# Attention unit: value products ahead of the carried-state matmuls, second masks ahead of the chain of states

## The reference, cut to what matters

```
B, H, S, D = 4, 8, 768, 48
for t in range(S):
    state = alpha[:, :, t, :, None] * state + einsum('bhd,bhe->bhde', k[:, :, t], v[:, :, t])
    y[:, :, t] = einsum('bhd,bhde->bhe', q[:, :, t], state)
```

## Time and profile before

| | before |
|---|---|
| median of 3 runs | 848.24 us |
| lowest, highest | 847.78, 849.92 us |
| profiled execution: span from first to last instruction (its own whole time is not shown) | 845.8 us |
| mean granted TensorE clock in it | 0.976 |
| TensorE busy | 784.4 us, 93% |
| VectorE busy | 409.7 us, 48% |
| ScalarE busy | 255.1 us, 30% |
| GpSimd busy | 268.3 us, 32% |

### The profile page before, as it was taken

One profiled execution on the slowest core, in us unless ns is written; L12 is line 12 of the kernel. 1 busy time (PEld: TensorE's weight loads), 2 busy tenths in 40 slices (PEclk: granted clock), 3 DMA queues, 4 the chain that ended last, 5 costly groups with the idle time before them and its releaser, 6 DMA issues.

```text
span 845.8 us, 15211 instructions
## 1 busy us (share of the span) xinstructions
PE 784.4 (93%) x4644; PEld 670.4 (79%) x4645; DVE 409.7 (48%) x735; ACT 255.1 (30%) x555; POOL 268.3 (32%) x170
## 2 busy tenths in 40 slices
PE   2988898989938999999999999999999999999998
PEld 2766676767726999999999987688888888888887
DVE  6788888888567334343333423433333333333322
ACT  5344636346232222222222222332222212122110
POOL 3245434352013745671826757410000001000000
PEclk9799999999878999999999999999999999999999
DMA  9966887845065814533325010210101101000001
GB/s 143 250 94 86 139 105 128 102 62 106 1 230 179 331 48 178 180 118 121 133 100 195 28 40 29 85 29 19 37 19 39 38 19 47 10 27 9 9 20 47
DMA packets 128881, 75.74 MB, mean 90 GB/s; under 512 B 102648, under 2 KB 122112, under 8 KB 128832
## 3 DMA queue, kind: packets, MB, share of 16 engines
q1 hardware_dynamic: 119632, 54.88, 30.0%
q0 software_dynamic: 3328, 10.23, 3.8%
q10 hardware_dynamic: 5872, 10.03, 3.2%
HBM read 59.00 MB, written 16.12 MB: 89 GB/s over the span
## 4 chain that ended last, share of the span: by engine, by line
PE 83%; DVE 11%; issue 2%; SPq 2%; DMA 1%; ACT 0%; POOL 0%; DVEq 0%; ACTq 0%
PE bank L1334 62%; DVE UA L834 4%; PE bank L1226 3%; DVE A L789 3%; PE bank L1136 3%; PE bank L1370 3%; PE bank L1196 2%; PE bank L1216 2%; PE bank L1166 2%; PE bank L1219 2%; SPq L300 2%; PE bank L1183 1%; PE bank L1320 1%; DVE UA L827 1%; PE bank L1406 1%
## 5 line engine op out<-in xcount | busy, mean ns | idle before, releaser
L465 POOL TENSOR_TENSOR wsp<-raw,wsp 128x1536 f32 x28 | 103.8, 3729 | 93.1 <-DVE wsp L1028 93.1
L1334 PE MATMUL bank<-yh,mh 128*128 128x512 f32 x324 | 128.3, 396 | 0.6 <-ACT yh L720 0.6
L1334 PE MATMUL bank<-yh,ml 128*128 128x512 f32 x324 | 126.5, 390 | 0.0
L1334 PE MATMUL bank<-yl,mh 128*128 128x512 f32 x324 | 91.3, 390 | 0.0
L1334 PE MATMUL bank<-wsp,xh 128*128 (+1 forms) x324 | 85.3, 399 | 3.7 <-issue 3.1
L1334 PE MATMUL bank<-wsp,hTh 128*128 x432 | 81.5, 340 | 1.1 <-ACT hTh L677 1.1
L506 POOL DMA_INDIRECT yg<-expert_rows,pos_i x24 | 24.7, 1029 | 171.8 <-ACT ygs L714 164.9
L1334 PEld LDWEIGHTS bank<-wsp,hTh 128*128 128x128 f32 x432 | 73.6, 188 | 1.3 <-issue 1.3
L1334 PEld LDWEIGHTS bank<-wsp,xh 128*128 128x128 f32 x324 | 58.9, 188 | 16.2 <-issue 4.0
L1098 DVE TENSOR_TENSOR t<-bank,tm 128x512 f32<-128x512 f32 x36 | 24.9, 692 | 96.5 <-PE bank L1334 96.5
L1334 PEld LDWEIGHTS bank<-yl,mh 128*128 128x128 f32 x324 | 60.9, 188 | 12.9
(11 more groups left out here) (197 smaller groups left out, 1394.8 us busy)
## 6 DMA issues: line engine op xcount, KB each, us to landing
raw<-in_moe_w SPq DMA_DIRECT2D x16, 1536.0 KB, 8.1
expert_rows<-ye ACTq DMA_DIRECT2D x27, 192.0 KB, 2.2
nat<-in_alpha SPq DMA_DIRECT2D x32, 144.0 KB, 3.1
nat<-in_k SPq DMA_DIRECT2D x32, 144.0 KB, 3.8
nat<-in_q SPq DMA_DIRECT2D x32, 144.0 KB, 4.3
vt<-in_v SPq DMA_DIRECT2D x32, 144.0 KB, 4.6
attention_rows<-xc SPq DMA_DIRECT2D x4, 1152.0 KB, 6.0
out<-oo SPq DMA_DIRECT2D x24, 192.0 KB, 1.9
```

What stands on the lines that cost most here:

```text
L465: g.tensor_tensor(wsp[:, ds(to, 1), 1, n, part], raw[:, n:n + 1, part], wsp[:, ds(to, 1), 0, n, part].bitcast(f32), ALU.subtract).then_inc ...
L1334: last = mm(o, x, y, start=(n == 0), stop=(n == len(todo) - 1))
```

## The change: value products, then carried states; second masks, then the chain

On TensorE all value products of a half are issued together (first half, then second half), each half behind its waits for masks and the keys' scaling. Then the five state matmuls follow, for chunks 1 to 5, each with its own wait, and add to what lies in PSUM. `pe_Y` is signalled behind the matmuls of chunk 2 and of chunk 5. On VectorE the two second masks are issued between the scans and the state products; they leave the chain.

```diff
@@ states (VectorE) @@
                 d.scalar_tensor_tensor(UA[j % 2][:, c, :], UA[j % 2][:, c - 1, :],
                                        A[j][:, P * c + P - 1:P * c + P], UA[j % 2][:, c, :],
                                        ALU.mult, ALU.add).then_inc(dve_st, 1)
-                if c <= 2:
-
-                    mask(u, j, 1, c - 1)
@@ step (VectorE) @@
             if base + j + 2 < NU:
                 scans(u + 2, (j + 2) % UPB)
+            for hd in range(2):
+                mask(u, j, 1, hd)
             states(u, j)
@@ unit (TensorE) @@
+            out = lambda cc: bank[2 + cc // HC][:, P * (cc % HC):P * (cc % HC) + P]
             for h in range(2):
                 if more:
                     pe.wait_ge(dve_kp, CR + 2 * (u + 1) + h + 1)
                 else:
                     pe.wait_ge(act_yT, CR + 2 * (u - 1) + h + 1)
                 pe.wait_ge(dve_S, CR + 4 * u + 2 * h + 2)
-                for c in range(HC):
-                    cc = HC * h + c
-                    o = bank[2 + h][:, P * c:P * c + P]
-                    if cc:
-
-                        pe.wait_ge(*((dve_UA, CR + u + 1) if cc == 1 else (dve_st, CR + 4 * u + cc - 1)))
-                        mm(o, UA[j % 2][:, cc - 1, :], qp[j % 2][:, P * cc:P * cc + P],
-                           start=True, stop=False, skip_group_check=True)
+
+                for cc in range(HC * h, HC * h + HC):
                     for hd in range(2):
-                        last = mm(o[HL * hd:HL * hd + HL], vt[j][:, cc, hd, :], Sm[j % 2][:, hd, cc, :],
-                                  start=not cc, stop=True, skip_group_check=True)
-                last.then_inc(pe_Y, 1)
+                        mm(out(cc)[HL * hd:HL * hd + HL], vt[j][:, cc, hd, :], Sm[j % 2][:, hd, cc, :],
+                           start=(cc == HC * h), stop=(cc == 0), skip_group_check=True)
+            for cc in range(1, CH):
+                pe.wait_ge(*((dve_UA, CR + u + 1) if cc == 1 else (dve_st, CR + 4 * u + cc - 1)))
+                last = mm(out(cc), UA[j % 2][:, cc - 1, :], qp[j % 2][:, P * cc:P * cc + P],
+                          start=False, stop=True, skip_group_check=True)
+                if cc in (HC - 1, CH - 1):
+                    last.then_inc(pe_Y, 1)
```

## The result

The changed kernel takes 869.47 us (median of 4 runs, 869.06 to 870.93), the kernel before 848.55 in the same comparison: ratio 1.0239, interval 1.0216 to 1.0262, so 20.9 us slower. The profiled execution has a span of 869.2 us and took 870.93.

What follows compares the result with a forecast made beforehand. VectorE's state chain, held by GpSimd's products, was taken to set when 11 of 16 attention units end. Terms 6.0 - 0.4 + 13.4 = +19.0 us on 848.2 gave 867.2 us, range 853 to 877.

Steps and rivals of the forecast that it cites:

- the third hold: VectorE's fourth state also held, by GpSimd's L420, in units 1 to 11 except 4 and 8: +0.67 us each, +6.0.
- the falls of the clock: TensorE's waits in attention lie together, so its clock falls in each of nine units, 1.67 us a fall: +13.4 us.
- Values first: TensorE in attention: 2.2 us of value work before the chain, none behind the last state; alone 0.37 us gained a unit.
- Masks first and the tie: VectorE's second state starts at 129.33, 0.02 us behind GpSimd's L407 (129.31), so it was taken as held.
- The bound from the row of 198.55: Kernel before: a state starting at 198.45, 0.10 us ahead of L407 at 198.55, gets through.
- the guess that a state could be caught after it has started: VectorE's free state could still be held by a GpSimd product up to some 0.2 us after its start.
- Units that were costed at nothing: Attention units with squares (three), unit 13 and the last two: change of 0 us.
- in the three units with squares no third state is held: Units where ScalarE first does squares: TensorE gains next to nothing, L1226 waits for ScalarE's copies: 0 us.
- The clock that stays: States held in attention, but TensorE's clock falls no further: +5.6 us, 853.8 us; chance 0.15.
- The second state getting through: Second state passes L407, two states held as before, 11 units gain 0.37 us each: 844.2 us; chance 0.15.
- the third rival: Second state passes but TensorE's clock falls more often: 848 us with two or three falls, 854 with six; chance within a shared 0.08.
- That the order does nothing: TensorE is the bound in attention, so the changed order has no effect: 848 us; chance within a shared 0.08.

Runs made afterwards that it cites:

- experiments 1 to 3: Changed kernel with, in turn, filler matmuls in TensorE's waits (850.11 us), GpSimd's L407 behind the four chained states (826.9), only weight products L420 and L422 behind them (858.81).
- experiment 4: Each half alone against the kernel before: value products first, masks still in the chain, 836.29 us; masks first, TensorE in the old order, 882.82 us.
- the two kernels with fillers: Filler matmuls put into TensorE's waits for states: in the changed kernel 850.11 us, in the kernel before 849.0 us.
- experiment 5: Changed kernel with GpSimd's L407 waiting for the first chained state of two units earlier, 854.94 us, or for the third, 825.04 us.
- experiment 6: Filler matmuls in TensorE's waits in the kernel before, 849.0 us; and in the changed kernel with L420 and L422 behind the states, 847.3 us.
- experiment 3: Changed kernel with only GpSimd's weight products L420 and L422 waiting for the fourth chained state: 858.81 us, ratio 1.0091.

## Why the prediction was right, point by point

**The forecast** was 867.2, the median 869.47. Both terms are the ones forecast, the third hold and the falls of the clock, and experiments 1 to 3 show each apart. That the number came within 2.3 us is partly luck: misses of several microseconds, below, cancel.

**Values first**: the value products do cover the wait for L829, and behind the last state one product remains. Alone it shortens the unit by 0.42 us (0.37 forecast). The 24 value products take 1.89 us, not 2.2, so the first wait came out longer than laid out: 1.48, 0.78 and 0.56 us, forecast 1.1, 0.85 and 0.62. That the masks bring no new wait holds in the steady units only; in unit 1 it is 1.54 us, in units 12 to 15 between 0.27 and 1.08.

**Masks first and the tie**: the second state was laid out 0.02 us behind L407, and in the nine units of the forecast it starts 0.01 to 0.02 us behind and is held, for 1.94 us; the third for 1.23, the fourth, behind L420, for 1.01. Unit 0 gets through with 0.13 us ahead of L407, as forecast. The bound from the row of 198.55 (0.10 us ahead passes) and the guess that a state could be caught after it has started hold too: 0.04 us ahead is held. One reading in the prediction has no support in the row that it names: that masks are not held. At 128.28 no GpSimd product runs. The trace of experiment 4 (values first alone) does show it: a mask that starts at 44.88, inside L407 (44.77, 1.86 us), takes 0.55 us.

**The third hold**: 0.67 us forecast, 0.61 measured between the two kernels with fillers.

**The clock**: this term was mis-sized. A fall was priced at 1.67 us, from unit 9. The nine units of the changed kernel are 15.78 to 17.50 us apart, on the mean of the eight behind unit 1 16.43, and with the clock up 14.26, so a unit's falls cost 2.2 us: 1.5 in units 5 and 9, in which the clock is low about as long as in unit 9 of before, 2.2 to 2.6 in the other six, in which it is low twice as long. The sum over the nine units is 23.4 us against the 19.4 forecast (9 x 2.34 - 1.67): 9 x 0.61 = 5.5 for the third hold, the other 17.9 for the clock, where 13.4 were forecast.

**Units that were costed at nothing**: units 4 and 8 kept their 12.3 us. Unit 12 did not: 14.19 instead of 12.32. The step "in the three units with squares no third state is held" is literally true and misses that the chain as a whole is 0.24 us later; in the earlier trace rows the fourth state of unit 12 passed L407 with only 0.10 us to spare, and now it starts 0.14 behind it and takes 1.82 us. At the end, from the scans of unit 13 on, attention is 1.7 us shorter than before, and the start 0.5 plus 0.5 us: 23.4 + 1.9 - 1.7 - 1.0 = 22.6 us, which is what attention grew by between the two profiles (22.7). With 0.7 us behind attention the spans differ by 23.4. The profiled execution of the changed kernel was the slowest of its four (870.93, median 869.47). That of before was about its fastest: its span is 845.8, and a span here lies 1.7 us under its execution's time (869.2 and 870.93), so it took some 847.5 us (median 848.55). That is why the medians differ by 20.9 only.

**The rivals.** The clock that stays (853.8) is what the fillers made, and they took the kernel's own earlier falls away too: 850.1. The second state getting through (844.2) is experiment 5, at 854.9: held states two as forecast, and 13.44 us between units where the clock stays up (13.27 by the forecast), but it falls in six of the nine, which was the third rival (854 with six falls). That the order does nothing is refuted by both halves alone.

**The rule of the Trainium skill** (TensorE: Matmul & The Clock Gate, "HAM oscillation"), that the clock falls when one wait of TensorE crosses the window over which its activity is watched, would have given +5.6 us. The traces differ: in its unit the fall at 128.03 has only the wait of 1.48 us before it. Another section of the same page, "A second HAM failure mode: psum-queue depth-cycling", tells of a kernel that cycles through PSUM banks, in which TensorE idles shortly between groups of matmuls so often that the clock swings between its two levels. These traces agree in so far as short waits go with falls; here the waits are for VectorE.

## What to carry to other kernels

An instruction that is moved out of a chain does not only shorten the chain, it moves all the rest of it against what other engines do: look at which of GpSimd's products each two-input VectorE instruction will meet at its new place, to 0.1 us. Where products of the two engines hold each other as here, it can pay to let GpSimd wait for the last link or the last but one of VectorE's chain: 26 us against the kernel before, for the change and one semaphore wait. And waits of TensorE that look short in the sum can cost twice, through its clock. Filler matmuls in the waits won that time back here; that must be measured for each kernel, since in the kernel before they cost about what they gave (experiment 6).

## What the runs showed of the hardware that was not expected

- A start of VectorE's state product 0.04 us ahead of GpSimd's product is still held (by 1.65 us, in four units of three runs); from 0.11 us ahead on it passed. No run has a start in between.
- One wait of 1.58 us and one of 0.78 with 2.2 us of matmuls between them left TensorE at its full clock in every steady unit (values first alone). With waits of 1.48 and 0.78 us and 0.42 us of work between them it fell in all nine units of experiment 3 and, with a third wait behind them, in all nine of the changed kernel. With waits of 1.34 and 0.78 us (experiment 5, first state) it fell in six of nine.
- The work between the waits can't be the whole reason. In units 3, 7 and 11 of experiment 3 the fall is recorded before the second wait begins, at 139.60 in unit 7 against 140.25. What decides stays open.
